# Attention, MoE and MLP on one core: one block for the 64-key tails of two query tiles

## The chip, the core and the metric

One core of a Trainium2 chip. The metric is the device time of one launch in microseconds (us), as the median of three runs.

## What is computed

Three layers follow one another, all in float32: attention of 4 batches x 8 heads x 576 tokens x 64, whose rows keep only scores within `tau` of the row's maximum; a mixture of 8 experts, one per token; and an MLP with a gated hidden layer. The change lies in the attention.

```python
scores = scale * np.matmul(q, k.transpose(0, 1, 3, 2))
thresh = np.max(scores, axis=-1, keepdims=True) - tau
scores = np.where(scores >= thresh, scores, -1000000000.0)
scores = scores - np.max(scores, axis=-1, keepdims=True)
attn = np.exp(scores)
attn = attn / (np.sum(attn, axis=-1, keepdims=True) + 1e-09)
return np.matmul(attn, v).astype(np.float32)
...
x = _moe_ref(x=x, **moe_kwargs)
return _moe2_ref(x=x, **moe2_kwargs)
```

## The kernel before

**Tiling.** A pair is one head of two batches ("side" 0 and 1), so there are 16 pairs, and two pairs make a quad (8 quads; quads 1 to 3 run as a hardware loop, the others are written out). 576 query rows are four tiles of 128 and a tail of 64. The two sides' tails share one tile, so a pair has U = 9 units: u = 0 to 3 are side 0's tiles, u = 4 (TAIL) is the shared tail tile, u = 5 to 8 are side 1's. That makes 144 units. A unit n has its scores made in step n and its probabilities transposed in step n + 5 (LAG), so step n of quad n // 18, with i = n % 18, does work for unit k = (i - 5) % 18.

**A step, engine by engine.** Each engine has its own program, in the same order of steps, and they meet at semaphores.

- PE: `transpose` (L1584). Four blocks of 128 keys of the unit's probabilities are transposed into `pt_ps` (L1587), after `probs_ready` (DVE's mask is done) and `keys_copied` (ACT has emptied the same four blocks of the step before). Then it waits for `turned_copied` (ACT has finished the whole step before), transposes the fifth block (64 keys and 64 zero columns, also L1587), and transposes q and k of a tile of the next pair (L1603). Then `score` (L1619): four matmuls of 288 keys (L1633), eight in u = 4. In steps u = 1 and u = 5, `values` (L1637) multiplies a side's transposed probabilities `pT` with v: 10 matmuls of 288 query columns with 64 columns of v as weights, on one half of the array or the other (L1646). In u = 3 and u = 7, `turn` (L1650) turns the result back.
- DVE: scales the scores and takes their row extreme (L1139), and later the mask with its row sum (L850). Also the write of x (L859).
- ACT: `copy_turned` (L1351) copies the four main blocks to `pT` (L1358, or L1349 for the unit of the shared tail tile), then the tail block (L1366), then q and k of the next pair (L1375; L1371 and L1373 in u = 4), and then it takes the exponentials of a unit (L1451) into one of six slots of `probs`. In u = 2 and u = 6 it first empties the values' bank (L1434, L1435).
- POOL: the threshold of a unit (L752), the split of q and k in two parts (L666, L668), and `swap` (L687), the copy of the keys with their halves exchanged (L692, L694).
- SP: loads of q, k, v (`load_v`, L489: six transfers a pair) and stores.

**Layout.** A slot of `probs` has 640 columns, of which the last 64 are zero and stay so. `qkT` holds q and k of a pair transposed, 1280 columns each, and the scores read side `s`'s keys from column 576 x `s`. Side 0's values read v in five blocks of 128 keys, the last with 64 zero rows; side 1's v has its tail first.

At L1598 to L1600, before:

```python
wait(pe, turned_copied, m)
if with_probs:
    mm = transpose_probs(TAIL)
```

`wait` puts a semaphore wait ahead of the next instruction. `wait_apart` (L450), where the value lies in a register (in the loop), makes the wait an instruction of its own that also counts up a semaphore; with a constant it is the same as `wait`.

## Time and profile before

| | us |
|---|---|
| three runs | 990.2, 990.82, 991.25 |
| median | 990.82 |
| the profiled execution, its own time | 988.91 |
| its span, first to last instruction | 986.9 |
| mean granted clock of PE | 0.997 |
| attention part | about 10 to 335 us of the span |

In the profile PE is the matmul engine, PEld its weight loads, DVE VectorE, ACT ScalarE, POOL GpSimd, SP SyncE. A group of instructions is given by its line, engine, operation and tiles, then how many, their busy time, the mean length in ns and the idle time of the engine just before them with what ended it. A timeline row has the start, the length, the engine and line, and how many instructions are merged in it. The length of a matmul's record is not its cost: matmuls overlap, and the distance of their starts is what one costs. Semaphore waits have no rows there.

### The profile page before, as it was taken

The page shows a single profiled execution, that of the slowest core. Times are in us where ns is not written, and L with a number is a line of the kernel's source. Part 1 is how long each engine was busy: PE and PEld are TensorE (multiplying, and loading weights), DVE is VectorE, ACT ScalarE, POOL GpSimd, SP SyncE. Part 2 cuts the span into 40 slices and gives each one's busy share as a digit, 9 for nine tenths or more (in the row PEclk, how much of TensorE's full clock was granted, in tenths as well). Part 3 has the DMA queues.
Part 4 walks back from the last instruction along what each step waited for, and adds up shares of the span by engine and source line. Part 5 has one row for each costly group of instructions (what it writes and reads, how often), then busy time and mean ns, then how long its engine had stood idle before and what let it go on. Part 6 is the DMA issues. An engine that isn't in the chain of part 4 may idle for free.

```text
span 986.9 us, 19143 instructions
## 1 busy us (share of the span) xinstructions
PE 963.0 (98%) x6541; PEld 865.4 (88%) x6542; DVE 497.7 (50%) x1141; ACT 448.4 (45%) x1047; POOL 271.8 (28%) x391
## 2 busy tenths in 40 slices
PE   5999999999999999999999999999999999999996
PEld 5787878787878899999999999899999999999995
DVE  6888888988889775122215245423222222222221
ACT  5877888787888514121124254322222222222222
POOL 6765666576666112111222000010010100100101
PEclk9999999999999999999999999999999999999998
DMA  3233222222344128311113442100100101000000
GB/s 80 54 60 76 48 60 64 65 54 63 93 113 122 47 87 277 108 43 43 43 44 126 160 139 64 54 33 1 33 32 0 64 0 32 32 0 0 33 1 33
DMA packets 106066, 61.10 MB, mean 62 GB/s; under 512 B 86525, under 2 KB 94747, under 8 KB 106011
## 3 DMA queue, kind: packets, MB, share of 16 engines
q1 hardware_dynamic: 95355, 44.37, 16.6%
q0 software_dynamic: 4160, 10.51, 3.4%
q10 hardware_dynamic: 6496, 5.54, 1.7%
q8 instruction: 29, 0.48, 0.2%
q14 instruction: 26, 0.21, 0.1%
HBM read 45.68 MB, written 14.70 MB: 61 GB/s over the span
## 4 chain that ended last, share of the span: by engine, by line
PE 92%; DVE 3%; issue 2%; ACT 1%; POOL 1%; DMA 0%; SPq 0%; ACTq 0%; POOLq 0%; DVEq 0%
PE s_ps L1867 20%; PE s_ps L1839 13%; PE s_ps L1701 11%; PE pt_ps L1587 9%; PE s_ps L1633 9%; PE o_ps L1646 8%; PE pt_ps L1839 6%; PE misc L1786 5%; PE o_ps L1786 5%; PE pt_ps L1603 2%; PE misc L1673 1%; PE pt_ps L1693 1%; PE misc L1663 1%; PE misc L1667 1%; DMA qk<-in_k_dram 0%
## 5 line engine op out<-in xcount | busy, mean ns | idle before, releaser
L1327 DVE TENSOR_TENSOR g<-s_ps,sig 128x384 f32<-128x384 f32 x96 | 53.5, 557 | 277.1 <-ACT sig L1558 277.1
L1558 ACT ACTIVATE sig<-s_ps 128x384 f32<-128x384 f32 x96 | 47.2, 492 | 271.4 <-PE s_ps L1867 271.4
L1139 DVE TENSOR_SCALAR_CACHE_REDUCE scores<-s_ps,taus 128x576 f32<-128x576 f32 x144 | 117.6, 817 | 42.0 <-PE s_ps L1633 25.7
L850 DVE SCALAR_TENSOR_TENSOR probs_and_slivers<-scores,thresh,probs_and_slivers 128x576 f32<-128x576 f32 x144 | 133.7, 929 | 0.0
L806 POOL DMA_INDIRECT out_dram<-out_sb,table x18 | 17.8, 990 | 417.6 <-ACT out_sb L1533 414.6
L1867 PE MATMUL s_ps<-yT_high,w_in_high 128*128 (+1 forms) x384 | 129.4, 337 | 0.3 <-issue 0.2
L1867 PE MATMUL s_ps<-yT_high,w_in_low 128*128 (+1 forms) x384 | 129.5, 337 | 0.0
L1867 PE MATMUL s_ps<-yT_low,w_in_high 128*128 (+1 forms) x384 | 128.9, 336 | 0.0
L1451 ACT ACTIVATE probs_and_slivers<-scores,row_low 128x576 f32<-128x576 f32 x144 | 116.0, 806 | 5.6 <-DVE scores L1139 4.1
L1587 PE MATMUL pt_ps<-ident,probs_and_slivers 128*128 128x128 f32 x720 | 106.1, 278 | 3.8 <-ACT pT L1349 1.0
L752 POOL TENSOR_TENSOR thresh<-row_low,taus 128x1 f32<-128x1 f32 x144 | 80.7, 562 | 96.8 <-DVE scores L1139 86.3
L1587 PEld LDWEIGHTS pt_ps<-ident,probs_and_slivers 128*128 128x128 f32 x720 | 79.4, 140 | 28.8 <-issue 18.9
L1633 PE MATMUL s_ps<-qkT 128*128 128x288 f32 x320 | 99.1, 327 | 2.0 <-POOL k_swap L694 1.6
L1701 PE MATMUL s_ps<-xT_high,w_high 128*128 128x256 f32 x320 | 91.3, 285 | 1.0 <-issue 1.0
L1701 PE MATMUL s_ps<-xT_low,w_high 128*128 128x256 f32 x320 | 90.5, 283 | 0.0
L1701 PE MATMUL s_ps<-xT_high,w_low 128*128 128x256 f32 x320 | 90.5, 283 | 0.0
L1633 PE MATMUL s_ps<-k_swap,qkT 128*128 128x288 f32 x320 | 88.7, 293 | 0.0
L1646 PE MATMUL o_ps<-pT,vv 128*64 128x288 f32 x640 | 84.7, 411 | 0.0
L1358 ACT COPY pT<-pt_ps 128x512 f32<-128x512 f32 x128 | 76.2, 596 | 9.7 <-PE pt_ps L1587 6.0
L1867 PEld LDWEIGHTS s_ps<-yT_high,w_in_high 128*128 128x128 f32 x384 | 72.2, 188 | 5.1 <-issue 1.0
L1839 PE MATMUL s_ps<-w_out_high,g_low 128*128 128x512 f32 x192 | 76.2, 397 | 0.0
L1839 PE MATMUL s_ps<-w_out_low,g_high 128*128 128x512 f32 x192 | 75.8, 395 | 0.0
(284 smaller groups left out, 2200.4 us busy)
## 6 DMA issues: line engine op xcount, KB each, us to landing
w_raw<-in_moe_w_dram SPq DMA_DIRECT2D x24, 512.0 KB, 4.3
yT_dram<-tile_yT ACTq DMA_DIRECT2D x10, 512.0 KB, 3.1
qk<-in_q_dram SPq DMA_DIRECT2D x32, 128.0 KB, 2.3
x_dram<-xs SPq DMA_DIRECT2D x32, 128.0 KB, 2.2
w_in_raw<-in_moe_w_in_dram SPq DMA_DIRECT2D x4, 1024.0 KB, 5.4
w_out_raw<-in_moe_w_out_dram SPq DMA_DIRECT2D x16, 256.0 KB, 2.6
qk<-in_k_dram SPq DMA_DIRECT2D x30, 128.0 KB, 2.4
next_yT<-yT_dram SPq DMA_DIRECT2D x5, 768.0 KB, 4.3
```

The costliest lines, as they stand in the source:

```text
L752: pool.tensor_tensor(thresh[:, j, u:u + 1], row_low[:, j, u:u + 1], taus[:, 4:5], ALU.add).then_inc(thresh_ready, 1)
L850: dve.scalar_tensor_tensor(out=probs[:, i % PROB_SLOTS, 0:SEQ], in0=scores[:, i % SCORE_SLOTS], scalar=thresh[:, j, u:u + 1], in1=probs[:, ...
L1139: dve.tensor_scalar(scores[:, i % SCORE_SLOTS].rearrange("p (c n) -> p c n", c=2), s_ps[i % 2][:, :, 0:HALF], taus[:, 3:4], None, ALU.mult ...
L1358: act.copy(pT[:, 0:TAIL, column(v):column(v) + P], pt_ps[:, 0:TAIL]).then_inc(keys_copied, 1)
L1451: act.activation(probs[:, k % PROB_SLOTS, 0:SEQ], scores[:, k % SCORE_SLOTS], ACT.Exp, bias=row_low[:, k // U, k % U:k % U + 1], scale=-1. ...
L1587: return pe.transpose(pt_ps[:, block], probs[:, k % PROB_SLOTS, block * P:(block + 1) * P], ident[:])
L1633: mm = pe.matmul(s_ps[i % 2][:, c, 0:HALF], qkT[j][:, 0, q_tile * P:(q_tile + 1) * P], keys[:, first:first + HALF], start=(at == 0), stop= ...
L1646: mm = pe.matmul(o_ps[lo:lo + DH, 0:HALF], vv[j][:, side, block], pT[:, block, at:at + HALF], start=(block == 0), stop=(block == TPB - 1))
L1701: mm = pe.matmul(hT_ps[f // 2][:, f % 2 * T:(f % 2 + 1) * T], w_part[:, a, f * P:(f + 1) * P], x_part[:, a], start=(a == 0 and part == 0), ...
L1786: mm = pe.matmul(yT_ps[d // 2][:, d % 2 * T:(d % 2 + 1) * T], w_part[:, f, d * P:(d + 1) * P], h_part[:, f], start=(at == 0 and part == 0) ...
L1839: mm = pe.matmul(mlp_y_ps[i], g_part[:, f % GT, at], w_part[:, f, :], start=(f == 0 and part == 0), stop=(f == FB2 - 1 and part == 2))
L1867: mm = pe.matmul(mlp_h_ps[f % 2], w_part[:, a, f * P:(f + 1) * P], y_part[:, bass.ds(c % 2 * DB + a, 1)].rearrange("p a b -> p (a b)"), st ...
```

## The change

Two units, an even one and the odd one behind it, have their tails transposed in one block.

- A slot of `probs` has 576 columns, and no zeros. Even units keep their 64 tail keys last, odd units first: the scores of an odd unit start 64 columns earlier, in a copy of the keys whose tail stands both before and after the 512 main keys (`keys_of`, 640 columns per side; `tails_of` are the two added copies of the tail, which ACT writes in u = 4). So the tails of an even and the next odd unit lie side by side, and one 128-column transpose takes both. `k_swap` has 640 columns per side as well.
- `tail_group`, `tail_closes` and `tail_block` say which units share a block. Of the 18 units of a quad, {0,1}, {2,3}, {6,7}, {10,11}, {12,13}, {14,15}, {16,17} share one, and 4, 5, 8, 9 have one each (a transpose of 64 weight columns). The transpose and ACT's copy to the new tile `pT_tail` are made in the step of the last unit of the group. In the steps without q and k to transpose (from step 135 on), the tail is transposed and copied in every step.
- Values: eight matmuls of 288 columns for the four main blocks, then for the tail four of 128 columns (one per unit) and two of 32 columns (the shared tail tile), with v's tail rows in either the upper or the lower half of a 128-row block whose other half is zero. v is loaded with the tail twice.
- PE waits for `turned_copied` with `wait_apart`.
- ACT's wait before the exponentials is for one count more of `turned`. Some memsets are added or moved at the start.

```diff
@@ constants and tiles
+    KEYS_AT = 2 * SPAD
+    SIDE_KEYS = SEQ + LAST
...
-        qkT = [put(f"qkT{b}", [P, 2, 2 * SPAD], F32R) for b in range(2)]
-        k_swap = [put(f"k_swap{b}", [P, 2 * SEQ], F32R) for b in range(2)]
+        qkT = [put(f"qkT{b}", [P, 2, KEYS_AT + LAST], F32R) for b in range(2)]
+        k_swap = [put(f"k_swap{b}", [P, 2 * SIDE_KEYS], F32R) for b in range(2)]
...
-        pT = put("pT", [P, TPB, 2 * SEQ])
-        vv = [put("vv0", [P, 2, TPB, DH])]
+        pT = put("pT", [P, TAIL, 2 * SEQ])
+        pT_tail = put("pT_tail", [P, TPB + 1, P])
+        vv = [put("vv0", [P, 2, TPB + 1, DH])]
...
+        def tail_group(k):
+            first = k // U * U
+            units = [x for x in (k - k % 2, k - k % 2 + 1) if first <= x < first + U
+                     and not (k // U == 0 and x in (TAIL, TAIL + 1))]
+            return units if k in units else [k]
+        def tail_closes(k):
+            return k == tail_group(k)[-1]
...
+        def tail_half(k):
+            group = tail_group(k)
+            return 1 if len(group) == 2 and k == group[1] else 0
+        def tail_parts(k):
+            return slice(0, P) if tail_closes(k) and len(tail_group(k)) == 2 else slice(0, LAST)
+        def keys_of(j):
+            return qkT[j][:].rearrange("p c n -> p (c n)")[:, KEYS_AT:KEYS_AT + 2 * SIDE_KEYS]
+        def tails_of(j):
+            return keys_of(j).rearrange("p (g q) -> p g q", q=LAST)[:, 0:2 * SIDE_KEYS // LAST:2 * SIDE_KEYS // LAST - 1]
@@ load_v
+                for side, seq in ((0, one), (1, two)):
+                    sp.dma_start(vv[j][:, side, 0:TAIL], seq[0:SEQ - LAST].rearrange("(t p) d -> p t d", p=P)
+                                 ).then_inc(v_loaded[j], 16)
+                    for half in range(2):
+                        sp.dma_start(vv[j][half * LAST:(half + 1) * LAST, side, TAIL + half], seq[SEQ - LAST:]
+                                     ).then_inc(v_loaded[j], 16)
@@ swap (POOL)
-                cols = slice(side * SEQ, (side + 1) * SEQ)
+                cols = slice(side * SIDE_KEYS, (side + 1) * SIDE_KEYS)
@@ DVE, start
-            dve.memset(o_slivers[:, 2 * LAST:], 0.0).then_inc(pads_cleared, 1)
+            dve.memset(o_slivers[:], 0.0).then_inc(pads_cleared, 1)
             for b in range(2):
                 dve.memset(vv[b][LAST:P, :, TAIL], 0.0).then_inc(pads_cleared, 1)
+                dve.memset(vv[b][0:LAST, :, TAIL + 1], 0.0).then_inc(pads_cleared, 1)
+            dve.memset(pT_tail[LAST:P], 0.0).then_inc(pads_cleared, 1)
@@ copy_turned (ACT)
+                with_tails = with_probs and (tail_closes(k) or not with_qk)
...
-                if with_probs:
-                    if v == TAIL:
-                        ins = copy_slivers(TAIL, TPB)
-                    else:
-                        ins = act.copy(pT[:, TAIL, column(v):column(v) + P], pt_ps[:, TAIL])
+                if with_tails:
+                    ins = act.copy(pT_tail[tail_parts(k), tail_block(k)], pt_ps[tail_parts(k), TAIL])
...
+                        act.copy(tails_of(tj), pt_ps[:, QK_AT + 1].rearrange("p (o q) -> p o q", o=2))
                         ins = act.copy(qkT[tj][:, 1, at], pt_ps[:, QK_AT + 1])
@@ step (ACT)
-                        wait(act, turned, n + U - 1)
+                        wait(act, turned, n + U)
@@ ACT, start
+            act.copy(tails_of(0), first_t[1].rearrange("p (o q) -> p o q", o=2)).then_inc(first_keys_copied, 1)
+            act.wait_ge(first_keys_copied, 3)
+            act.copy(k_swap[0][0:DH, 0:SIDE_KEYS], keys_of(0)[DH:P, 0:SIDE_KEYS]).then_inc(turned_copied, TPB)
@@ transpose (PE)
+                def transpose_tails():
+                    if tail_closes(k) and len(tail_group(k)) == 2:
+                        here = slot * SEQ
+                        tails = probs[:].rearrange("p s n -> p (s n)")[:, here - LAST:here + LAST]
+                    else:
+                        first = 0 if slot % 2 else TAIL * P
+                        tails = probs[:, slot, first:first + LAST]
+                    return pe.transpose(pt_ps[tail_parts(k), TAIL], tails, ident[:])
...
-                wait(pe, turned_copied, m)
-                if with_probs:
-                    mm = transpose_probs(TAIL)
+                wait_apart(pe, turned_copied, m)
+                if with_tails:
+                    mm = transpose_tails()
@@ score (PE)
+                tail_last = LAST if i % 2 == 0 else 0
...
-                        first = side * SEQ + c * HALF
+                        first = side * SIDE_KEYS + tail_last + c * HALF
@@ values (PE)
-                for block in range(TPB):
+                for block in range(TAIL):
                     for lo, at in ((0, side * SEQ), (DH, side * SEQ + HALF)):
-                        mm = pe.matmul(o_ps[lo:lo + DH, 0:HALF], vv[j][:, side, block], pT[:, block, at:at + HALF],
-                                       start=(block == 0), stop=(block == TPB - 1))
+                        pe.matmul(o_ps[lo:lo + DH, 0:HALF], vv[j][:, side, block], pT[:, block, at:at + HALF],
+                                  start=(block == 0), stop=False)
+                for of in range(TAIL // 2):
+                    for h in range(2):
+                        k = j * U + side * TPB + h * (TAIL // 2) + of
+                        pe.matmul(o_ps[h * DH:(h + 1) * DH, of * P:(of + 1) * P], vv[j][:, side, TAIL + tail_half(k)],
+                                  pT_tail[:, tail_block(k)], start=False, stop=False)
+                for h in range(2):
+                    k, here = j * U + TAIL, h * LAST + side * SLIVER
+                    mm = pe.matmul(o_ps[h * DH:(h + 1) * DH, HALF - SLIVER:HALF], vv[j][:, side, TAIL + tail_half(k)],
+                                   pT_tail[:, tail_block(k), here:here + SLIVER], start=False, stop=True)
```

## Rows read from the trace of the kernel before

**Rows 1.** The page, busy time, share of the span and instructions by engine.

```profile
PE 963.0 (98%) x6541; PEld 865.4 (88%) x6542; DVE 497.7 (50%) x1141; ACT 448.4 (45%) x1047; POOL 271.8 (28%) x391
```

**Rows 2.** Stage 60 to 330 us: busy time by engine, clock, DMA share, GB/s.

```profile
60.00:330.00 270.00, 266.94 (x2130) 219.77 (x2129) 234.24 (x603) 221.99 (x576) 170.30 (x255) 1.00 0.32 77
```

**Rows 3.** Timeline, one side's values (step u = 5): PE, then its first loads.

```profile
154.47 0.29 PE L1633 MATMUL s_ps<-k_swap,qkT 128*128 128x288 f32 x1
154.69 2.65 PE L1646 MATMUL o_ps<-pT,vv 128*64 128x288 f32 x20
...
156.93 0.41 PE L1646 MATMUL o_ps<-pT,vv 128*64 128x288 f32 x2
157.27 0.77 PE L1587 MATMUL pt_ps<-ident,probs_and_slivers 128*128 128x128 f32 x5
...
154.69 0.14 PEld L1646 LDWEIGHTS o_ps<-pT,vv 128*64 128x64 f32 x2 [0.16 <-issue]
```

**Rows 4.** Groups by line, 60 to 300 us: busy us, mean ns | idle before.

```profile
L1139 DVE TENSOR_SCALAR_CACHE_REDUCE scores<-s_ps,taus 128x576 f32<-128x576 f32 x110 | 89.9, 817 | 31.5 <-PE s_ps L1633 18.8 <-ACT probs_and_slivers L1451 4.4 <-POOL thresh L752 4.0
L1587 PE MATMUL pt_ps<-ident,probs_and_slivers 128*128 128x128 f32 x554 | 81.5, 278 | 1.7 <-ACT pT L1349 0.5
...
L1633 PEld LDWEIGHTS s_ps<-qkT 128*128 128x128 f32 x244 | 45.7, 187 | 0.1
...
L1646 PEld LDWEIGHTS o_ps<-pT,vv 128*64 128x64 f32 x480 | 32.4, 137 | 22.8 <-issue 3.1 <-ACT pT L1358 0.8
...
L1615 PE MATMUL pt_ps<-early_slot_tok,early_row_hot 128*128 128x4 f32 x9 | 1.1, 249 | 0.0
```

**Rows 5.** Timeline, steps u = 7, 8, 0 and the start of 1: PE, then ACT.

```profile
158.69 0.74 PE L1587 MATMUL pt_ps<-ident,probs_and_slivers 128*128 128x128 f32 x5
159.19 0.37 PE L1603 MATMUL pt_ps<-ident_r,qk_parts 128*128 128x128 f32 x2
...
160.93 0.71 PE L1587 MATMUL pt_ps<-ident,probs_and_slivers 128*128 128x128 f32 x5
...
162.06 0.29 PE L1633 MATMUL s_ps<-k_swap,qkT 128*128 128x288 f32 x1
162.30 0.74 PE L1587 MATMUL pt_ps<-ident,probs_and_slivers 128*128 128x128 f32 x5
...
163.47 0.29 PE L1633 MATMUL s_ps<-k_swap,qkT 128*128 128x288 f32 x1
163.89 0.30 PE L1587 MATMUL pt_ps<-ident,probs_and_slivers 128*128 128x128 f32 x1
...
161.57 0.59 ACT L1358 COPY pT<-pt_ps 128x512 f32<-128x512 f32 x1 [0.31 <-PE pt_ps L1587]
162.05 0.27 ACT L1366 COPY pT<-pt_ps 128x128 f32<-128x128 f32 x1
162.21 0.39 ACT L1375 CAST qkT<-pt_ps 128x256 fp32r<-128x256 f32 x1
162.47 0.80 ACT L1451 ACTIVATE probs_and_slivers<-scores,row_low 128x576 f32<-128x576 f32 x1
163.15 0.76 ACT L1349 COPY pT<-pt_ps 128x512 f32<-128x512 f32 x2
```

**Rows 6.** Timeline, PE, two places outside the usual step.

```profile
223.97 0.27 PE L1611 MATMUL pt_ps<-ident,gates 128*9 128x128 f32 x1
223.99 0.38 PE L1633 MATMUL s_ps<-qkT 128*128 128x288 f32 x1
...
272.02 1.13 PE L1615 MATMUL pt_ps<-early_slot_tok,early_row_hot 128*128 128x4 f32 x9
```

**Rows 7.** Timeline, the start: PE and DVE.

```profile
10.14 0.37 PE L1633 MATMUL s_ps<-qkT 128*128 128x288 f32 x1 [0.41 <-ACT k_swap L1462]
...
17.77 0.40 PE L1633 MATMUL s_ps<-qkT 128*128 128x288 f32 x1 [1.55 <-POOL k_swap L694]
...
4.62 0.49 DVE L824 CAST qk_parts<-qk 128x640 fp32r<-128x640 f32 x1 [1.17 <-DMA qk<-in_k_dram]
```

More of the change, by code:

```diff
@@ L417, in attention_moe_mlp_kernel, with tail_block @@
         A_ROWS, T_ROWS, B_ROWS = slice(0, TAIL), slice(TAIL, TAIL + 1), slice(TAIL + 1, U)
+        assert U % 2 == 1 and PROB_SLOTS % 2 == 0 and STEPS % PROB_SLOTS == 0
+        def tail_group(k):
[5 more added lines that the diff above has]
+            return k == tail_group(k)[-1]
+        def tail_block(k):
+            first = k // U * U
+            return len({tuple(tail_group(x)) for x in range(first, k + 1)}) - 1
+        def tail_half(k):
[7 more added lines that the diff above has]
+            return keys_of(j).rearrange("p (g q) -> p g q", q=LAST)[:, 0:2 * SIDE_KEYS // LAST:2 * SIDE_KEYS // LAST - 1]
         def column(v):
@@ L1581, in _ @@
         def _(pe):
-            pe.wait_ge(consts, 3)
+            pe.wait_ge(consts, 2)
             def transpose(m, ahead, k, tj, tu, with_probs, with_qk, extra=None):
+                slot = k % PROB_SLOTS
+                main_at = LAST if slot % 2 else 0
                 def transpose_probs(block):
-                    return pe.transpose(pt_ps[:, block], probs[:, k % PROB_SLOTS, block * P:(block + 1) * P], ident[:])
+                    first = main_at + block * P
+                    return pe.transpose(pt_ps[:, block], probs[:, slot, first:first + P], ident[:])
+                def transpose_tails():
[6 more added lines that the diff above has]
+                    return pe.transpose(pt_ps[tail_parts(k), TAIL], tails, ident[:])
+                with_tails = with_probs and (tail_closes(k) or not with_qk)
                 if with_probs:
@@ L1626, in score @@
                 sides = ((TAIL, 0), (U, 1)) if u == TAIL else ((u, 0 if u < TAIL else 1),)
-                passes = [(q_tile, side, keys) for q_tile, side in sides for keys in (qkT[j][:, 1], k_swap[j])]
+                passes = [(q_tile, side, keys) for q_tile, side in sides for keys in (keys_of(j), k_swap[j])]
+                tail_last = LAST if i % 2 == 0 else 0
                 wait(pe, low_ready, n - 1)
```

57 lines of the change are left out of this document (26 added, 31 removed).

## The prediction

> **What bounds the kernel now.** I read the whole page first: PE is busy 98% of the span, DVE 50%, ACT 45% [rows 1]; in the attention part, which ends near 330 us, DVE and ACT are the busier ones that one must suspect too. The stage view settles their size: from 60 to 330 us PE 266.94 of 270, DVE 234.24, ACT 221.99, with PE's clock at 1.00, its 2.4 GHz level [rows 2]. DMA's share is 0.32, so nothing in the loads binds. A busy PE is not a PE without waits, so the third view is the timeline around the values and around a pair's end, steps u = 7 to 1 [rows 3, 5]. One step of PE is four main transposes of L1587, the tail transpose, two of L1603, four score matmuls of L1633, in u = 4 four more, in u = 1 and 5 the values (L1646), in u = 3 and 7 the turning back.
>
> Two kinds of steps must be told apart. **Long steps** (u = 1, 3, 4, 5, 7): PE's own work is longer than anything it waits for; step u = 7 runs from 158.69 to 160.93 with matmuls close together throughout [rows 5]. **Short steps** (u = 0, 2, 6, 8): the four main transposes write the one set of pt_ps blocks, and the next step's may start only when ACT has copied them. In step u = 8 that copy starts at 161.57 and ends at 162.16, and the next transposes start at 162.30, 0.24 after the last score matmul's start (162.06), where 0.13 to 0.14 is what one costs without a wait [rows 5]. So a short step already waits 0.1 us. Step u = 0 waits more: its main copy comes from L1349 and starts at 163.15, because ACT goes through tail copy (162.05), q and k copy (162.21), exp (162.47), and the next transposes start at 163.89, 0.42 after the last score [rows 5].
>
> From 60 to 300 us DVE scans 110 units (L1139), so a unit lasts 240/110 = 2.18 us and a pair of nine 19.6. Before them DVE sat idle 31.5 us, and PE ended most of that, 18.8 [rows 4]: DVE is second, and PE waits for it nowhere in the steps I looked at.
>
> **Term 1, tail transposes.** One transpose costs 0.11 us: five of L1587 last 0.71, less one record's 0.28, over four intervals [rows 4, 5]. Units of a quad (18): groups close after k = 1, 3, 7, 11, 13, 15, 17 and 4, 5, 8, 9 stay single, so 7 of 18 tail transposes go. They go from steps i = 5, 7, 11, 15, 17 and, a quad later, 1 and 3. In the drain (n from 135) nothing is left out, which keeps 5 (k = 6, 10, 12, 14, 16 of the last quad): 8 x 7 - 5 = 51 of 144 go. Of these 21 (i = 11, 15, 17 of seven quads) fall into short steps, which end with the copy of the main blocks, and that copy hangs on the fourth main transpose, not the fifth: I cost them at nothing. 30 (i = 5, 7 of eight quads, 1, 3 of seven) fall into long steps: 30 x 0.11 = 3.3 us gained.
>
> In quads 1 to 3, which run in a loop, the wait for turned_copied becomes an instruction of its own. In steps i = 1, 3, 7 it is late: ACT's q and k copy of the step before ends 0.30 after the new step's first transpose (162.21 + 0.39 = 162.60 against 162.30) [rows 5], and from a copy's end to the matmul that waited for it pass 0.14 us (162.16 to 162.30). So L1603 can start 0.44 after the step's first transpose, where it started 0.50 after (158.69 to 159.19): in these nine steps 0.06 is gained and not 0.11. That takes 9 x 0.05 = 0.5 us off term 1. Queued behind this wait are L1603 and the scores; who waits for them (ACT, DVE) has slack, see above. Where the wait is already met it is taken ahead by PE's sequencer, so I price it at nothing; if it were not, 54 such waits at 0.1 are 5.4 us.
>
> **Term 2, ACT.** 51 tail copies (L1366, the next copy starts 0.16 later: 162.05 to 162.21) go, and 15 copies of both halves of the tail keys come in at u = 4, where the values of u = 5 hide them (PE's next need of a copy is over 3 us off). ACT's time counts only before step u = 0's main copy. At i = 17 the copy goes (7 quads), at i = 8 (k = 3 closes a pair) it stays: 7 x 0.16 = 1.1 us gained. At most 0.19 could come, then the fourth transpose ends last.
>
> **Term 3, values.** One side was 20 instructions (10 calls, two each) of 288 columns; two on the two halves of the array run side by side: 2.65 less 0.41 is 2.24 from the first pair's start to the tenth's, 0.249 a pair [rows 3], the first with the array still filling. 288 columns twice at 2.4 GHz are 0.240, and I take 0.242. The two tail pairs (0.48) become four pairs of 128 columns and two of 32. The columns are the same 576. By columns a 128 pair takes 0.242 x 128/288 = 0.108. A 32 pair would be 0.027, but a load of 64 weight columns takes longer: loads of 64 columns last 137 ns, of 128 columns 187 [rows 4], so 64 columns are 0.05; nine matmuls of only 4 columns behind 128-column loads follow at (1.13 - 0.25)/8 = 0.11 [rows 6], which fits two times 0.05. So the first 32 pair costs about 0.06; of the last one only 0.03 counts, since what follows waits for the array to empty in both kernels. Sum 0.43 + 0.06 + 0.03 = 0.52, 0.04 more; with some refill I take 0.05: 32 sides x 0.05 = 1.6 us lost. Bounds: 0.04 below; above, if the loads of the two halves go one after the other, 4 x 0.12 + 2 x 0.12 = 0.72, 0.23 more or 7.4 us; if every one of the 12 instructions cost 0.11, 1.32, 26.8 us. Two loads of 0.14 lie in 0.14 [rows 3], so they do run side by side; I take the low one.
>
> By the Trainium skill, TensorEngine Tiling, section Instruction Overhead, every matmul carries about 60 cycles, and one of few columns costs as much as one of 60. At 2.4 GHz that would be 8 x 0.025 x 32 = 6.4 us for the eight instructions more a side, and with it in place of my 1.6 the sum would be 2.8 us slower. The trace disagrees for the 288-column pair: of 0.249 the columns take 0.240, which leaves no room for two times 0.025.
>
> **Term 4, start and the rest.** Before the first scores ACT does one copy more (about 0.2) and a swap of 640 columns for 576; PE waits for just that (L1462, [rows 7]). But the first steps then wait on POOL (L694) up to 17.77 [rows 7], whose swaps grow by a ninth. I take 0.3 us lost, bounds 0 and 0.7. Later no wait of PE for a swap stands among the stage's rows that I read. Added memsets of DVE end before its 1.17 us wait for the loads does [rows 7]. v is loaded with six transfers a pair as before, one ninth more rows in SP's queue at 0.32 DMA share: nothing. The stage behind attention is untouched and keeps its length.
>
> **Sum.** -3.3 + 0.5 - 1.1 + 1.6 + 0.3 = -2.0 us. The profiled execution took 988.91 (span 986.9), 1.9 under the median of 990.82. I forecast 988.8 against that median. A measurement of this kernel can tell about 0.2%, 2 us.
>
> **Rivals.** (a) More carries over: the 21 hidden transposes count too, since a shorter step lets scores and hence everything behind start earlier, and values cost nothing more. Then -5.6 - 1.1 + 0.3 = -6.4 us, 984.4. Against it: the copy wait in step u = 8, which the tail has no part in. 0.17 for something between -3.5 and this.
> (b) Slower, **array mode**: the single tails are now transposes of 64 weight columns. Rows show that going from the scores to the half-array values costs 0.22 instead of 0.13 (154.47 to 154.69), and back 0.34 instead of 0.24 (156.93 to 157.27) [rows 3]. If 64-column transposes switch likewise, 32 of them plus 5 of the drain, at 0.19 each, are 7.0 us: 5.0 us slower, 995.8. It decides as soon as over 9 of them pay. The Trainium skill, TensorEngine Tiling, section Key Properties, has the rule that changing tiling mode drains TensorE. Against it: one transpose of 9 columns (L1611) stands between L1603 and L1633 with starts 223.97 and 223.99, no drain at either side [rows 6]. By that rule, the trace agrees for the values and not for a narrow transpose. 0.08.
> (c) Values bound by serial loads or a cost for each instruction: 7.4 for 1.6 us, 3.8 us slower, 994.6. 0.10. The full 26.8 us, 0.02.
> (d) No saving at all, because long steps too turn into waits for ACT: +1.9 us. 0.08.
>
> **Numbers.** My case (between -3.5 and 0) has 0.55, and nearly half of it lies beyond 2 us: faster 0.25 + 0.17 = 0.42. Slower 0.08 + 0.10 + 0.02 and a fifth of (d) is 0.22; the rest, 0.36, is within. The likeliest case's own range is 987.3 to 990.8. The range reaches to most of (a) and to (c): 985.3 to 995.
>
> **What would show it.** Step u = 7 and u = 3 of unrolled quads 0.11 shorter, in quads 1 to 3 only 0.06; steps 11, 15, 17 as long as before; step 0 shorter by 0.16, step 9 not; values plus the way out 2.62 to 2.65 instead of 2.58; gaps around 64-column transposes as around others; first scores at 10.4 instead of 10.14. The forecast is wrong if short steps shrink too, if a 32-column pair takes over 0.1, or if gaps of 0.1 stand at the single tails.

## The result and the profile after

| comparison | kernel before, us (runs) | changed kernel, us (runs) | ratio, 95% interval | long step n = 146 in the profile |
|---|---|---|---|---|
| first | 990.83 (20) | 993.46 (20) | 1.0024, 1.0017 to 1.0031 | yes |
| A | 990.38 (33) | 989.12 (11) | 0.9984, 0.9975 to 0.9993 | no |
| B | 990.89 (28) | 993.80 (7) | 1.0028, 1.0017 to 1.0039 | yes |
| C | 990.20 (33) | 988.37 (11) | 0.9984, 0.9975 to 0.9993 | no |
| D | 990.53 (21) | 993.16 (11) | 1.0024, 1.0015 to 1.0033 | yes |
| E | 990.53 (21) | 988.21 (11) | 0.9984, 0.9975 to 0.9993 | no |

The first comparison is the result that the forecast is held against: 0.24% slower, 2.6 us, where 2.0 us faster was forecast. A to E are the later ones, with the same two kernels. The medians of the changed kernel are 988 to 989 or 993 to 994, and its single runs do not overlap either: without the long step none is above 990.02 (A, E), with it none is below 991.25 (D). A and B ran on the same chip. The median of the kernel before stays at 990.2 to 990.9 throughout.

The page of the changed kernel in the first comparison, busy time by engine (its own time 992.25 us, span 990.3, mean granted clock 0.995); it answers to [rows 1]:

```profile
PE 963.7 (97%) x6746; PEld 877.1 (89%) x6747; DVE 503.0 (51%) x1144; ACT 444.3 (45%) x1012; POOL 273.9 (28%) x390
```

The sums say little. ACT has 35 instructions fewer and 4.1 us less, PE 205 more at the same busy time, since a side of values now takes 28 instructions for 20. The change in PE's busy share comes from the span. So the next view is the stages, 60 to 330 us as in [rows 2], then the place around 326 us, still the first comparison:

```profile
60.00:330.00 270.00, 263.83 (x2283) 225.57 (x2283) 236.96 (x603) 216.77 (x542) 173.89 (x255) 1.00 0.33 79
...
326.00:328.00 2.00, 0.37 (x4) 0.40 (x5) 0.00 (x0) 1.09 (x3) 0.00 (x0) 1.00 0.20 76
328.00:332.00 4.00, 4.00 (x23) 4.00 (x22) 1.28 (x2) 2.18 (x4) 0.00 (x0) 0.57 0.02 4
```

PE is busy 3.1 us less than in [rows 2] though it has more to do: it waits. It stood still just before 328 us, and from 328 to 332 the granted clock is 0.57 of full, so for most of these 4 us (3.4 us by the trace's clock records) it was at the 1.2 GHz level. The timeline of that place, PE and then ACT:

```profile
320.97 2.16 PE L1707 MATMUL o_ps<-pT,vv 128*64 128x288 f32 x16
322.96 0.61 PE L1712 MATMUL o_ps<-pT_tail,vv 128*64 128x128 f32 x8
323.39 0.26 PE L1716 MATMUL o_ps<-pT_tail,vv 128*64 128x32 f32 x4
323.58 0.66 PE L1637 MATMUL pt_ps<-ident,probs 128*128 128x128 f32 x4
324.07 0.27 PE L1646 MATMUL pt_ps<-ident,probs 128*128 128x128 f32 x1
327.63 0.63 PE L1637 MATMUL pt_ps<-ident,probs 128*128 128x128 f32 x4 [3.29 <-ACT pT L1400]
...
328.60 0.41 PE L1771 MATMUL s_ps<-xT_high,w_low 128*128 128x256 f32 x1
328.81 0.41 PE L1771 MATMUL s_ps<-xT_high,w_high 128*128 128x256 f32 x1
...
322.00 1.06 ACT L1448 CAST xT_high<-s_ps 128x512 fp32r<-128x512 f32 x2
325.46 0.37 ACT L1478 COPY oT<-o_ps 128x256 f32<-128x256 f32 x1 [2.39 <-remote]
325.73 0.19 ACT L1479 COPY o_slivers<-o_ps 128x32 f32<-128x32 f32 x1
326.90 0.59 ACT L1400 COPY pT<-pt_ps 128x512 f32<-128x512 f32 x1 [0.98 <-remote]
```

This is the end of step n = 146, the third behind the last score (146 and 147 have no scores between their transposes, and the expectations below call the two together "step n = 146"). PE's last matmul of the values ends in the records at 323.39 + 0.26 = 323.65, but ACT's copy that waits for it starts at 325.46, 1.8 us later; the four transposes end at 324.24, and ACT's copy of them starts at 326.90, 2.7 us later. Both copies are marked "remote": the profile finds no instruction whose end released them. The trace also keeps the time of each semaphore update, and it says where the delay lies: the update by the last matmul of the values stands at 325.44, 1.79 us behind that matmul's record and 0.02 ahead of ACT's copy; in E it stands at 323.75, 0.03 behind it. So ACT is not slow to see it. Either the update was held up, or the matmuls themselves ran later than their records, whose ends are modelled. PE itself then waits 3.29 us. In the kernel before, the same place has a wait of 0.66 us:

```profile
325.80 0.74 PE L1587 MATMUL pt_ps<-ident,probs_and_slivers 128*128 128x128 f32 x5 [0.66 <-ACT pT L1358]
```

Its matmuls of L1701 start 0.12 us apart where those of L1771 in the changed kernel start 0.21 us apart. In E the changed kernel has no such gap:

```profile
323.46 0.26 PE L1716 MATMUL o_ps<-pT_tail,vv 128*64 128x32 f32 x4
323.65 0.66 PE L1637 MATMUL pt_ps<-ident,probs 128*128 128x128 f32 x4
324.15 0.27 PE L1646 MATMUL pt_ps<-ident,probs 128*128 128x128 f32 x1
325.07 0.63 PE L1637 MATMUL pt_ps<-ident,probs 128*128 128x128 f32 x4 [0.66 <-ACT pT L1400]
325.54 0.27 PE L1646 MATMUL pt_ps<-ident,probs 128*64 128x128 f32 x1
325.57 0.36 PE L1771 MATMUL s_ps<-xT_high,w_high 128*128 128x256 f32 x1
325.77 0.28 PE L1771 MATMUL s_ps<-xT_low,w_high 128*128 128x256 f32 x1
325.89 0.28 PE L1771 MATMUL s_ps<-xT_high,w_low 128*128 128x256 f32 x1
...
323.77 0.37 ACT L1478 COPY oT<-o_ps 128x256 f32<-128x256 f32 x1 [0.64 <-PE o_ps L1716]
```

**Where the time is, by stretches.** A stretch runs from the first transpose (L1587, now L1637) of one step to that of another, read from PE's timeline. E has both kernels side by side, each at a mean clock of 0.998: spans 987.3 (before) and 986.3 (after).

| stretch | before, us | change in E | change by the forecast |
|---|---|---|---|
| start to the end of quad 0 | 45.38 | -0.03 | +0.18 |
| quads 1 to 3, i = 0 to 8 | 3 x 19.6 | -0.90 | -1.05 |
| quads 4 to 7, i = 0 to 8 | 4 x 19.6 | -1.93 | -2.0 |
| quads 1 to 6, i = 9 to 17 | 118.5 | +1.00 | +0.6 |
| quad 7, i = 9 to 17 (drain) | 18.68 | +0.74 | +0.1 |
| n = 144 to 147 | 8.75 | 0.00 | +0.05 |
| the rest, to the end | 658.6 | +0.09 | +0.05 |

In sum -1.03; 0.35 of the +1.00 is a single step, i = 13 of quad 1, which takes 1.80 us before and anything from 1.81 to 2.55 in the executions of the changed kernel. In the first comparison the same table has +0.35 up to n = 9 for a start 0.58 later than in the profile of before, and +4.18 in the row n = 144 to 147 (12.93 instead of 8.75); the other rows agree with E within 0.4 us. Of the 4.18, 2.63 are step 146, with the wait, and 1.54 step 147, at the lower clock. So one place costs four times what the change brings.

### The profile page after: what moved, and what is told of

Same layout as the page of the kernel before. It is cut to its first block, busy times and chain, and to the rows that moved or that the text cites. A ratio compares the mean times of both kernels' runs of the same rounds, so it can differ in the third digit from the quotient of the medians.

```text
span 990.3 us, 19577 instructions
## 1 busy us (share of the span) xinstructions
PE 963.7 (97%) x6746; PEld 877.1 (89%) x6747; DVE 503.0 (51%) x1144; ACT 444.3 (45%) x1012; POOL 273.9 (28%) x390
## 4 chain that ended last, share of the span: by engine, by line
PE 88%; DVE 4%; issue 3%; ACT 2%; POOL 1%; DMA 0%; another core or an unknown queue 0%; SPq 0%; ACTq 0%; DVEq 0%; POOLq 0%
PE s_ps L1937 20%; PE s_ps L1909 13%; PE s_ps L1771 11%; PE s_ps L1694 8%; PE pt_ps L1637 7%; PE pt_ps L1909 6%; PE o_ps L1707 6%; PE misc L1856 5%; PE o_ps L1856 5%; PE pt_ps L1663 1%; PE o_ps L1712 1%; DVE probs L891 1%; PE pt_ps L1646 1%; PE pt_ps L1763 1%; PE misc L1733 1%
## 5 line engine op out<-in xcount | busy, mean ns | idle before, releaser
L891 DVE SCALAR_TENSOR_TENSOR probs<-scores,thresh,probs 128x576 f32<-128x576 f32 x144 | 135.1, 939 | 0.0
L1495 ACT ACTIVATE probs<-scores,row_low 128x576 f32<-128x576 f32 x144 | 114.3, 794 | 10.5 <-DVE scores L1180 7.9
L1637 PE MATMUL pt_ps<-ident,probs 128*128 128x128 f32 x576 | 90.0, 279 | 6.6 <-ACT pT L1400 3.5
L1771 PE MATMUL s_ps<-xT_high,w_high 128*128 128x256 f32 x320 | 91.8, 287 | 1.0 <-issue 1.0
L1771 PE MATMUL s_ps<-xT_low,w_high 128*128 128x256 f32 x320 | 91.1, 285 | 0.0
L1771 PE MATMUL s_ps<-xT_high,w_low 128*128 128x256 f32 x320 | 91.1, 285 | 0.0
L1637 PEld LDWEIGHTS pt_ps<-ident,probs 128*128 128x128 f32 x576 | 63.5, 141 | 19.9 <-issue 12.5
L1937 PEld LDWEIGHTS s_ps<-yT_low,w_in_high 128*128 128x128 f32 x384 | 72.1, 188 | 4.0
```

Source lines behind the costliest of these rows:

```text
L891: dve.scalar_tensor_tensor(out=probs[:, i % PROB_SLOTS, 0:SEQ], in0=scores[:, i % SCORE_SLOTS], scalar=thresh[:, j, u:u + 1], in1=probs[:, ...
L1495: act.activation(probs[:, k % PROB_SLOTS, 0:SEQ], scores[:, k % SCORE_SLOTS], ACT.Exp, bias=row_low[:, k // U, k % U:k % U + 1], scale=-1. ...
L1637: return pe.transpose(pt_ps[:, block], probs[:, slot, first:first + P], ident[:])
L1771: mm = pe.matmul(hT_ps[f // 2][:, f % 2 * T:(f % 2 + 1) * T], w_part[:, a, f * P:(f + 1) * P], x_part[:, a], start=(a == 0 and part == 0), ...
L1937: mm = pe.matmul(mlp_h_ps[f % 2], w_part[:, a, f * P:(f + 1) * P], y_part[:, bass.ds(c % 2 * DB + a, 1)].rearrange("p a b -> p (a b)"), st ...
```

## The experiments

### Repeats: is the slowdown a property of the kernel?

Both kernels once more, without an edit.

> The kernel before, unchanged. Ratio 1.000. In the one profile of the kernel after, PE runs 3.4 us at half clock around 14 us and again around 328 us, and none of that stands in the profile of before. Clock theory: the runs of before have a higher mean granted clock than the 0.990 to 0.996 of the kernel after, mostly 0.996 or more. Stall theory (the 3.3 us in which PE waits near 324 us is there in every run of the kernel after, whatever the clock): the clocks of before may be the same as those of after.

> The kernel after, unchanged. Ratio 1.002 to 1.003. Stall theory: PE's wait of about 3.3 us near 324 us stands in this profile too, and the last scores of attention come 0.5 to 1 us earlier than in the kernel before. Clock theory: the stall may be gone or elsewhere, but stretches at half clock stand near the start or between 310 and 345 us again, and each costs about 1 to 1.7 us.

Measured in A: 990.50 (ratio 1.0002, 0.9993 to 1.0011) and 989.12 (0.9984). From the scan of unit 9 to that of unit 143 ("first to last scan" in the expectations) it took 292.16 and 291.10 us, in the first comparison 292.03 and 290.93. The changed kernel has 290.9 to 291.5 there in all six of its profiles, with and without the long step, so the difference of sign had to lie outside. Both theories behind e2 missed, for both said 1.002 to 1.003: there is no wait of 3.3 us in this profile, and the stretch at half clock near the start (10.2 us) stands in e1 as well; single runs in A have a mean clock of 0.992 to 0.998 for the changed kernel and 0.992 to 0.999 for the kernel before. It led to B, with the changed kernel and three variants:

> The changed kernel, unchanged. In the first comparison it took 993.46 us against 990.83, in the second 989.12 against 990.38, and the profiles of the two differ mainly at one place: in the first, step n = 146 (the third of those behind the last score) lasts 8.09 us, in the second 3.92. Theory A: the 4.2 us are a property of how the program lies in one comparison and not of its work. Then this run gives either about 993 with one step of 8 us near 324 us, or about 989 with 3.9 us there, with nothing between, and the kernel before stays at 990.4. Theory B: the long step is a chance of single executions. Then single times of this run spread from 988 to 994.

Measured: 993.80, and the profile has the long step. It is again all or nothing, and it was in all four kernels of B. In C:

> The changed kernel once more, as the control of this comparison. So far the long step n = 146 (8 us for 3.9, PE's releases 1.8 and 2.6 us behind its matmuls' records) stood in every kernel of two comparisons and in none of the third, so it is a property of a comparison: about 993 us with it or about 989 without, and steps 10 to 145 as before (first to last scan without it 1.1 us shorter than in the kernel before).

988.37, no long step in any of the four kernels. Theory A of these two holds as far as it goes: what is measured is one of two cases, and a comparison has one or the other.

### Which part comes with the long step?

e3, e10 and e14 bring back the tail transpose and ACT's copy in every step:

```diff
-                with_tails = with_probs and (tail_closes(k) or not with_qk)
+                with_tails = with_probs
```

> The kernel after, but every step transposes and copies a tail (an open group as 64 columns, as the last steps do). It brings back 51 transposes and 51 copies. By the prediction (3.3 - 0.5 + 1.1 us saved by them) this is 3.9 us slower than the kernel after, ratio 1.006 to 1.007 of before. If the saving never reached the end (it ends in a wait or a lower clock near 320 us), it is as slow as the kernel after, 1.002 to 1.003.

> The changed kernel with a tail transpose and its copy in every step. Theory A: the long step belongs to the values in pieces or to the changed order of work in the drain, so that this kernel has it whenever the control has: about 996 with it, 992.5 without. Theory B: the long step needs the lead that PE gains by the left out transposes; then this kernel is at 992.5 though the control is at 993. In either case odd and even steps i = 1, 3, 5, 7 are 0.11 us longer than the control's and i = 11, 15, 17 equal.

> The changed kernel with tail transposes and copies in every step. If the control has the long step: 996 if it comes with the values in pieces or the new layout, 992.3 if it needs the transposes that were left out. If the control has none: 992.3, as twice.

e4, e11 and e15 are the kernel before with nothing but the values' tail block in pieces:

```diff
-                for block in range(TPB):
+                for block in range(TAIL):
...
+                for first, wide in ((0, P), (P, P), (2 * P, SLIVER)):
+                    for lo, at in ((0, side * SEQ), (DH, side * SEQ + HALF)):
+                        mm = pe.matmul(o_ps[lo:lo + DH, first:first + wide], vv[j][:, side, TAIL],
+                                       pT[:, TAIL, at + first:at + first + wide], start=False, stop=(wide == SLIVER))
```

> The kernel before, with the tail block of the values made in pieces of 128, 128 and 32 columns in place of 288. By the prediction 32 x 0.05 = 1.6 us slower, ratio 1.0016. If the loads of the two halves go one after the other, 7.4 us, 1.0075. If the pieces shorten the way out of the array more than they cost, 0 or faster. The profile gives the distance from the last 288-column pair to the next step's first transpose: 0.84 us by the prediction (2.62 in place of 2.58 in all).

> The kernel before with the tail block of the values in pieces of 128, 128 and 32 columns. If the pieces (32-column matmuls ahead of a transpose) bring the long step about, it has one when the control has: about 996. If not, it stays at 991.8, 0.038 us a side or 1.2 us above the kernel before, which has shown no long step in any profile.

> The kernel before with the values' tail block in pieces. If the control has the long step and this one too (995.5), the pieces alone bring it. If the control has it and this one not (991.6), another part does. If the control has none: 991.6, as twice.

| | A | C | D (long step) |
|---|---|---|---|
| kernel before | 990.38 | 990.20 | 990.53 |
| changed kernel | 989.12 | 988.37 | 993.16 |
| tails in every step | 992.48 | 992.02 | 996.47 |
| before with pieces | 991.85 | 991.44 | 994.64 |

The control of D (e13, the changed kernel) was expected at about 993 us with the long step or 989 without, and has it. Two things follow. First, the terms can be read off: the 51 transposes and copies are worth 3.36, 3.65 and 3.31 us net, and the pieces cost 1.47 and 1.24. Net, because with a tail in every step PE loses its lead, and the late swap described below goes with it: step i = 4 of the looped quads is 1.80 again and i = 9 of the last quad 1.59. Second, in D the kernel before with the pieces alone has the long step as well, in the timeline of PE and then of ACT:

```profile
326.60 0.69 PE L1650 MATMUL o_ps<-pT,vv 128*64 128x128 f32 x12
327.22 0.76 PE L1587 MATMUL pt_ps<-ident,probs_and_slivers 128*128 128x128 f32 x5
331.26 0.74 PE L1587 MATMUL pt_ps<-ident,probs_and_slivers 128*128 128x128 f32 x5 [3.27 <-ACT pT L1358]
...
332.07 0.28 PE L1705 MATMUL s_ps<-xT_high,w_low 128*128 128x256 f32 x1
332.19 0.28 PE L1705 MATMUL s_ps<-xT_high,w_high 128*128 128x256 f32 x1
...
329.08 0.37 ACT L1434 COPY oT<-o_ps 128x256 f32<-128x256 f32 x1 [2.36 <-remote]
329.35 0.19 ACT L1435 COPY probs_and_slivers<-o_ps 128x32 f32<-128x32 f32 x1
330.53 0.59 ACT L1358 COPY pT<-pt_ps 128x512 f32<-128x512 f32 x1 [0.99 <-remote]
```

The same two late releases at the same place, without shared tail blocks, without 64-column transposes and with the old layout. So the long step does not need them, nor the lead that PE gains; e14, with a tail in every step, has it too. Here the clock stayed at 2.4 GHz (starts 0.12 apart), and the row n = 144 to 147 is 2.62 us longer. With the fall of the clock it is 3.7 to 4.8 us longer in the other eight profiles of the long step. In all nine, step 146 alone takes 4.02 to 4.07 us for 1.42, so the wait itself is worth some 2.6 us and the half clock behind it the rest. Whether the clock falls differs between executions; the engine had stood idle for 3.3 us in both cases.

The narrow matmuls ahead of the place were one suspect. e12 leaves out the two 32-column pairs of the very last side (so its output lacks the tail keys in the columns of the shared tail tile there):

> The changed kernel without the two 32-column pieces of the very last side (pair 15, side 1), so the columns of the shared tail tile lack the tail keys there. If these pieces are what delays the release behind the last values, then no long step here though the control has one: about 989. If the delay has nothing to do with them, equal to the control.

Measured in C: 988.75, but its control had no long step either, so this run tells nothing of it.

Last, the control that was missing: a copy of the kernel before in the place of the changed one.

> The kernel before, put in the place of the changed one. If the long step n = 146 belongs to the change, this kernel never has it: 990.5 us, ratio 1.000, whether the control e18 has it or not. If it belongs to the place in a comparison and not to the kernel, then this kernel has it when e18 has: about 994 us and a step of 7 to 8 us near 326 us.

> The changed kernel beside it: about 993 us with the long step or about 989 without. Only with it does this pair tell the two theories apart.

Measured in E: 989.60 (ratio 0.9996, 0.9987 to 1.0005) and 988.21. E had no long step, so this pair does not tell the two apart. Two statements are shown: the long step appeared in all nine profiles of kernels other than the kernel before that the first comparison, B and D have, and in none of the eight such of A, C and E, nor in the two copies of the kernel before in A and E; and the kernel before, timed beside them in every comparison, stayed within 990.2 to 990.9. Whether a mere copy of it would get the long step in a comparison like B was not measured, and what makes ACT's release late is open.

One more difference divides the same profiles, and it begins before the wait. The trace keeps a record for each completion of a transfer. Up to 300 us all twenty profiles have 5,109 to 5,111 of them. From 300 to 320.5 us, ahead of the wait, the nine with the long step have 178 to 223 and the eleven others 268 to 284; in all, 6,873 to 6,991 against 7,526 to 7,571, though the number of DMA packets differs by at most 3 for the same program. The page shows it as a transfer without a landing time, here first in the first comparison, then in E:

```profile
out_dram<-out_sb,table POOLq DMA_INDIRECT x18
out_dram<-out_sb,table POOLq DMA_INDIRECT x18, 2.7
```

All nine profiles with the long step have the first form of this line and the eleven others the second. Between 323.0 and 325.4 us of the first comparison records of semaphore updates by ACT and DVE are missing too, whose instructions are all there. So the long step comes together with lost records of semaphore events, and the first of these are lost some 10 us earlier. Whether one causes the other, or a third thing both, is not shown. That the recording itself holds the update back is a rival that nothing here excludes: every timed run has a span and a granted clock on record, and none without recording is there to compare.

### The late swap

The tables of step lengths showed losses that no term of the forecast has: i = 4 of the looped quads 1.93 us instead of 1.80, i = 13 of the last quad 2.00 instead of 1.60, i = 9 there 1.83 instead of 1.59. Timeline of E's changed kernel, PE, POOL and DVE, step i = 4 of quad 2:

```profile
93.10 0.60 PE L1637 MATMUL pt_ps<-ident,probs 128*128 128x128 f32 x4
93.53 0.27 PE L1646 MATMUL pt_ps<-ident,probs 128*128 128x128 f32 x1
93.56 0.37 PE L1663 MATMUL pt_ps<-ident_r,qk_parts 128*128 128x128 f32 x2
93.92 0.40 PE L1694 MATMUL s_ps<-qkT 128*128 128x288 f32 x1
...
91.78 0.72 POOL L732 CAST k_swap<-qkT 64x640 fp32r<-64x640 f32 x1 [0.33 <-ACT qkT L1419]
92.66 1.13 POOL L734 CAST k_swap<-qkT 64x640 fp32r<-64x640 f32 x1 [0.17 <-POOL k_swap L732]
...
93.13 0.69 DVE L1193 TENSOR_SCALAR row_sum_eps<-row_sum 128x9 f32<-128x9 f32 x1
```

The scores start 0.36 behind the first transpose of L1663 instead of 0.21: POOL's second copy ends at 92.66 + 1.13 = 93.79, and the scores, which wait for the swap, start 0.13 later. That copy took 1.13 us where its twin took 0.72, and DVE's small instruction beside it 0.69 where the one at 309.38 takes 0.16. In step i = 13 of quad 1 the profile of E names the swap itself as what ended PE's wait (in D, where that step takes 2.55 us, it names it with 0.55):

```profile
74.47 0.40 PE L1694 MATMUL s_ps<-qkT 128*128 128x288 f32 x1 [0.15 <-POOL k_swap L734]
```

Step i = 13 of the last quad, POOL, DVE and PE in the same order of places:

```profile
306.45 1.61 POOL L732 CAST k_swap<-qkT 64x640 fp32r<-64x640 f32 x1
308.12 0.72 POOL L734 CAST k_swap<-qkT 64x640 fp32r<-64x640 f32 x1
...
306.26 1.22 DVE L1126 TENSOR_TENSOR w_low<-w_raw,w_high 128x1024 fp32r<-128x1024 f32 x1
307.40 0.81 DVE L1180 TENSOR_SCALAR_CACHE_REDUCE scores<-s_ps,taus 128x576 f32<-128x576 f32 x1
308.13 1.31 DVE L891 SCALAR_TENSOR_TENSOR probs<-scores,thresh,probs 128x576 f32<-128x576 f32 x1
309.38 0.16 DVE L1193 TENSOR_SCALAR row_sum_eps<-row_sum 128x9 f32<-128x9 f32 x1
...
308.05 0.60 PE L1637 MATMUL pt_ps<-ident,probs 128*128 128x128 f32 x4
308.48 0.27 PE L1646 MATMUL pt_ps<-ident,probs 128*64 128x128 f32 x1
308.89 0.40 PE L1694 MATMUL s_ps<-qkT 128*128 128x288 f32 x1
```

The swap ends at 308.84 and the scores start at 308.89; without the wait they would start some 0.03 behind the tail's transpose, at 308.51. In the profile of before this swap ends at 309.61, 0.08 us ahead of the scores, which did not wait for it:

```profile
308.94 0.67 POOL L694 CAST k_swap<-qkT 64x576 fp32r<-64x576 f32 x1
309.69 0.38 PE L1633 MATMUL s_ps<-qkT 128*128 128x288 f32 x1
```

Since a waiting matmul starts 0.05 behind the swap in E, no more than 0.03 us of this was to spare. POOL's copy beside DVE's two-input instruction takes 1.61 us for 0.72, DVE's mask beside POOL's copy 1.31 us for its usual 0.81. The kernel before has the same meeting in this step (1.56 us for 0.67, and 1.21 for 0.81); what is new is that PE arrives earlier at the end of it. By the Trainium skill, SBUF — State Buffer, section "SBUF: two separate sides", GpSimd and a DVE instruction with two inputs in SBUF share one pair of ports that the first to start holds to its end; the trace agrees in the main, for POOL's copy started beside a DVE instruction that ran to 307.48 and ended 0.58 us behind it, where alone it takes 0.72. Three variants of the changed kernel in B, and one of them again in D:

```diff
@@ e6, e16: POOL, swap
-                wait_apart(pool, k_swapped, done + 1)
@@ e7: POOL, last quad
-                    if isinstance(quad, int) and quad == QUADS - 1 and i in (9, 14):
-                        at = (9, 14).index(i)
+                    if isinstance(quad, int) and quad == QUADS - 1 and i in (11, 14):
+                        at = (11, 14).index(i)
@@ e8: PE, transpose
-                wait_apart(pe, turned_copied, m)
+                (wait_apart if with_tails and len(tail_group(k)) == 1 else wait)(pe, turned_copied, m)
```

> The changed kernel without POOL's wait between the two copies of a swap. Theory: PE now meets the swap of the keys of side 1 in step i = 4 of the looped quads (1.93 us instead of 1.80) and in step i = 13 of the last quad (2.00 instead of 1.60), since the swap has 640 columns, starts later against PE, and is drawn out beside DVE. The wait costs 0.17 us between the copies, so i = 4 shrinks by 0.13, i = 13 by 0.17 to 0.4, in sum 0.6 to 0.8 us less than the changed kernel. Rival: those steps wait for DVE (its mask and reciprocals) or ACT, then they stay at 1.93 and 2.00 and the sum is 0.

> The changed kernel with POOL's scaling of the first gathered rows (1.57 us) moved from step i = 9 of the last quad to i = 11, behind the swap. Theory of the late swap: step i = 13 of the last quad goes from 2.00 back to 1.60, 0.4 us less; nothing else moves. Rival (DVE is what ends step i = 13): stays at 2.00. Either way step i = 9 of that quad stays at 1.83, because there ACT's exponentials wait for DVE's scan.

> The changed kernel, in which PE's wait for turned_copied is joined to the next instruction again, except ahead of a single tail's transpose. It differs in the looped quads alone. Theory of the prediction: a wait of its own that is already met costs nothing, one that is late costs 0.05 in i = 1, 3, 7. Then steps 3 and 7 go from 1.70 and 2.16 to 1.68 and 2.12 at most, 0.2 to 0.3 us in all. Rival: what holds these steps is ACT's copy and not the wait's form, so they stay as they are; 0.0 us.

> The changed kernel without the wait between the two copies of a swap. The steps i = 4 of the looped quads are 0.13 us shorter in two of three, and first to last scan 0.4 us shorter than the control's (290.56 against 290.93). So 0.3 to 0.4 us below the control, and, if the control is at 989, about 2 us below the kernel before: the fastest of all.

| | time, us | i = 4, quads 1, 2, 3 | i = 13, last quad | i = 3 and 7, looped |
|---|---|---|---|---|
| changed (B, e5) | 993.80 | 1.93, 1.81, 1.94 | 2.02 | 1.70, 2.15 |
| e6 | 992.89 | 1.80, 1.94, 1.80 | 2.01 | 1.70, 2.15 |
| e7 | 992.76 | 1.92, 1.99, 1.92 | 2.02 | 1.70, 2.15 |
| e8 | 993.29 | 1.95, 2.03, 1.99 | 2.02 | 1.68, 2.12 |
| changed (D, e13) | 993.16 | 1.92, 1.80, 1.93 | 2.00 | 1.70, 2.15 |
| e16 | 992.81 | 1.79, 1.92, 1.79 | 2.01 | 1.70, 2.15 |

e6 and e16: without the pause two of the three looped steps lose their 0.13 us, which is the swap shown as their bound there; the middle one, 1.81 and 1.80 in these two controls but 1.96 to 1.98 in the four other profiles of the changed kernel, takes 1.94 and 1.92. First to last scan is 290.56 and 290.63, against 291.50 and 291.44 in their own controls and 290.93 to 291.21 in the other four; most of the distance to the own controls is step i = 13 of quad 1 (1.84 and 1.85 for 2.54 and 2.55), which is as short in e7 and e8, with the pause, and is not counted. The last quad's step does not move: there the copy stands behind DVE and not behind the pause, so at most half of what was expected came. The medians, 0.9 and 0.35 us below their controls, are within what such a comparison can tell. e7: a miss, i = 13 stays at 2.02, since the swap starts behind the threshold of i = 10, and that behind DVE's scan, with or without the scaling. Its median is 1.0 below the control with no step of the profile to carry it, and is not counted. e8: the joined wait gives 0.02 and 0.03 in i = 3 and 7, about as expected, and 0.03 to 0.04 in i = 1, and step i = 4 takes them back (1.95 to 2.03): PE arrives earlier at the same swap. Apart from step i = 13 of quad 1 no other step moves by more than 0.02, so a wait of its own that is already met costs nothing that can be seen.

## Why the prediction was wrong

**The direction was wrong, and the step that failed is that the sum has no term for the last steps of attention, n = 144 to 147, beyond the 0.05 us of a side.** It puts them at nothing without a reason. In the first comparison they took 4.18 us more. The sentence that "the stage behind attention is untouched and keeps its length" held for what comes after them (658.6 us in both). No rival had it either: all four price the steps and values of the attention part. The views shown before the change have no sign of it, for the kernel before waits 0.66 us there. What the runs showed in its place: releases from PE to ACT that come 1.8 and 2.7 us late in some comparisons, in the kernel before with pieces alone as in the changed one, which cost 2.6 us, and in eight of nine profiles a clock that falls to 1.2 GHz behind PE's wait, for another 1.1 to 2.1. Why the releases are late stays open, and so does whether a mere copy of the kernel before would have them too. By the Trainium skill, TensorE: Matmul & The Clock Gate, "What's actually happening", the clock of an idle array is 1.2 GHz; the trace agrees in the first comparison, in B and in three of D's profiles, while in e15 no fall followed the same wait.

**Without the long step the number was about right, for reasons that were right in part.** Ratio 0.9984 three times is 1.6 us, the forecast was 2.0; the stretches of E add up to 1.0. That it came so close is in part luck, since terms 3 and 4 were put too high and the swap was left out.

- Term 1, unrolled quads: right. i = 3 is 1.68 for 1.79, i = 7 is 2.12 for 2.23, each 0.11 less. Looped quads: i = 3 is 1.70 and i = 7 2.15, 0.08 less, where 0.06 was said; the price of a wait that is met is 0, as said (e8).
- Steps 11, 15, 17 do not shrink: right. [Rows 5] has step u = 8 at 160.93 to 162.30, 1.37 long with its tail transpose; in E, without it, it is again 1.37 (160.97 to 162.34):

```profile
160.97 0.60 PE L1637 MATMUL pt_ps<-ident,probs 128*128 128x128 f32 x4
161.32 0.37 PE L1663 MATMUL pt_ps<-ident_r,qk_parts 128*128 128x128 f32 x2
...
162.34 0.63 PE L1637 MATMUL pt_ps<-ident,probs 128*128 128x128 f32 x4
162.80 0.27 PE L1646 MATMUL pt_ps<-ident,probs 128*128 128x128 f32 x1
```

- Term 2: step 0 is 1.52 for 1.68 in the looped quads (0.16, as said) and 1.47 for 1.59 in the others (0.12). Step 9 stays at 1.59, except in the last quad (1.83).
- Terms 1 and 2 together were put at 3.9 us; bringing the transposes and copies back costs 3.3 to 3.65, net of what the swap then gives back. That rules out rival (d), no saving at all, and since steps 11, 15 and 17 kept their length, rival (a) as well.
- Term 3: 0.05 a side was said; the step with a side is 0.04 longer (i = 10: 4.01 for 3.97), and side and way out take 2.61 (320.97 to 323.58) for 2.58. The pieces alone cost 1.24 and 1.47 for 1.6, and e4 has 0.86 us from the last 288-column pair to the next transpose where 0.84 was expected. Rival (c), 7.4 us, is out by that, and the second 32-column pair follows 0.03 behind the first.
- Rival (b), array mode, is out: in E's rows above, the 64-column transpose at 325.54 stands 0.47 behind the first of its four neighbours, the 128-column one at 324.15 stands 0.50 behind its first, and the matmul after the narrow one starts 0.03 later. (The prediction's count there is off: at 0.19 us each, 11 such transposes and not 9 turn a gain of 2.0 us into a loss.)
- Term 4: too high. In E the first scores start at 10.47 for 10.49 in the copy of the kernel before. The 10.14 of [rows 7] was an early start of that one execution, and a forecast of 10.4 from it was not worth its digit.
- What the sum lacked is about 1.3 us between n = 18 and 143 (E has -1.09 in the four rows for which it said -2.35). The swap alone has 1.2 us in E: 0.13, 0.18 and 0.13 in i = 4 of quads 1 to 3, 0.35 in i = 13 of quad 1, 0.40 in i = 13 of the last. "No wait of PE for a swap stands among the stage's rows that I read" was true of the kernel before, but how near the swap came was not measured (0.08 us in the last quad): it comes later against a PE that is ahead, has 640 columns, and is drawn out beside DVE. And in the last quad DVE is the bound, with scans 2.62 and 2.37 us apart (304.78, 307.40, 309.77 in E) against PE's short steps of 1.4 to 1.6, so there the lead of 0.48 us gained in i = 0 to 8 is handed back (0.74 lost in i = 9 to 17, of which the swap has 0.4 and DVE, through ACT's exponentials, 0.24).

So of the 3.3 to 3.65 us that the left out transposes and copies bring net, the pieces of the values take back 1.2 to 1.5, and the long step takes back more than all of it where it appears. The 1.2 us of the late swap are for the most part already taken off in that net figure; without them the change would bring about twice what it does (an estimate from the steps of E).

## What to carry to other kernels

When a saving is spread over many steps, look for the neighbour with the smallest margin (here POOL's swap, 0.08 us ahead in one place) and ask by how much the faster engine overtakes it; and cost the last stretch by itself, because another engine may bound it. A difference of 0.2% between two kernels is not settled by one comparison, however many runs it has: the 20 runs of the first all lay above the median of the kernel before, and three of five repeats came out on the other side with intervals that do not touch. Before a mechanism is sought for such a number, the two profiles are to be laid side by side by stretches, which here put 4.2 us into one place where the spans differ by 3.3. And where a wait has no releaser, look whether the records of the semaphores are complete before reasoning from them; here one in twelve of the completion records was missing.

## What was unexpected of the hardware

- Releases of PE that ACT gets 1.8 and 2.7 us after the record of the matmul that makes them, always at the same instruction, in every kernel of a comparison but the kernel before or in none, on the same chip. The transfers beside them run without them too (DMA share 0.48 from 320 to 326 us in both the first comparison and C), and the clock falls only behind them. What they come with is completion records that are missing from some 10 us earlier on.
- Behind a wait of 3.3 us the granted clock was at 1.2 GHz in eight profiles and stayed at 2.4 GHz in one (e15). The fall came at a price of 1.1 to 2.1 us on top of the 2.6 that the wait costs.
- 32-column matmuls into the two halves of the array cost 0.03 us a pair when they follow others. By the Trainium skill, TensorEngine Tiling (Array Packing), section Instruction Overhead, a matmul of few columns takes as long as one of 60. At 2.4 GHz that is an estimate of 0.025 us from the page's figure, and 0.05 for two in turn; the trace agrees with it only if the two halves overlap.
- POOL and DVE lengthen each other's instructions here by 0.5 to 0.9 us at a time (0.72 to 1.61, 0.81 to 1.31, 0.16 to 0.69), and did so in the kernel before.
